# A recurrent attention layer and two expert layers in one kernel: unit 2's outputs, a third hidden bank and wider products in the opening

## The reference

```python
for t in range(S):                     # per batch and head
    m_new = max(f[t] + m, i[t])
    C = exp(f[t] + m - m_new) * C + exp(i[t] - m_new) * outer(v[t], k[t])
    n = exp(f[t] + m - m_new) * n + exp(i[t] - m_new) * k[t]
    y[t] = sigmoid(o[t]) * (C @ q[t]) / max(abs(n @ q[t]), 1)
x = y as 1536 x 320
h = x @ w_in                           # 320 x 2048
g = where(h >= 1, h, where(h <= -1, 0, (h + 1)**2 / 4))
x = g @ w_out                          # 2048 x 320
P = softmax-like gate of x @ w_gate, 8 rounds of row and column scaling
out = sum over 8 experts e of P[:, e] * (max(x @ w1[e], 0) @ w2[e])
```

## Time and profile before

| | |
|---|---|
| median of 3 runs | 923.47 us (922.88 to 923.96) |
| the profiled execution | 923.94 us, of which its span 921.8 us |
| TensorE, matmul busy | 914.6 us, 99% |
| VectorE, ScalarE, GpSimd busy | 594.1, 464.6, 617.8 us |
| granted clock of TensorE, mean | 1.000 |

### The profile page before, as it was taken

The page is one execution under the profiler, slowest core; times in us unless marked ns, Lnnn a source line. Parts: engine busy times, 40 slices in busy tenths (PEclk is TensorE's granted clock), DMA queues, the critical chain, the costliest instruction groups (busy, mean ns, idle before and its releaser), DMA issues.

```text
span 921.8 us, 16392 instructions
## 1 busy us (share of the span) xinstructions
PE 914.6 (99%) x6091; PEld 902.2 (98%) x6091; DVE 594.1 (64%) x1130; ACT 464.6 (50%) x951; POOL 617.8 (67%) x642
## 2 busy tenths in 40 slices
PE   9999999999999999999999999999999999999998
PEld 7899999999999999999999999999999999999998
DVE  7665444447867888866666666666666666666665
ACT  4655545448864445454444445444445444445442
POOL 6963555454786666777777677767776777777652
PEclk9999999999999999999999999999999999999999
DMA  8904324001110111111111111111111111111102
GB/s 263 302 27 115 93 61 104 32 2 38 38 54 22 38 38 38 38 39 59 38 53 38 38 38 38 49 51 44 46 38 38 39 38 60 38 52 38 38 1 86
DMA packets 27599, 53.02 MB, mean 58 GB/s; under 512 B 2304, under 2 KB 15584, under 8 KB 27264
## 3 DMA queue, kind: packets, MB, share of 16 engines
q1 hardware_dynamic: 25984, 46.13, 17.2%
q10 hardware_dynamic: 1440, 5.77, 1.6%
q0 software_dynamic: 96, 0.07, 0.0%
HBM read 49.92 MB, written 2.04 MB: 56 GB/s over the span
## 4 chain that ended last, share of the span: by engine, by line
PE 64%; DVE 1%; issue 0%; ACT 0%; DVEq 0%
PE bank L1680 33%; PE bank L1657 30%; DVE acc L1291 0%; DVE prob L1262 0%; DVE rowsum L1260 0%; DVE prob L1272 0%; DVE h_lo L1308 0%; DVE c L1327 0%; DVE c L1317 0%; DVE acc L1295 0%; ACT h_hi L703 0%; PE bank L1628 0%; ACT h_hi L698 0%; DVE rowinv L1261 0%; DVE colinv L1270 0%
## 5 line engine op out<-in xcount | busy, mean ns | idle before, releaser
L1657 PE MATMUL bank<-xo,wu 128*128 128x384 f32 (+1 forms) x1792 | 377.5, 338 | 0.7 <-DVE s L1311 0.5
L1657 PEld LDWEIGHTS bank<-xo,wu 128*128 128x128 f32 (+1 forms) x1792 | 306.6, 188 | 1.4 <-DVE s L1311 0.7
L1295 DVE SCALAR_TENSOR_TENSOR acc<-bank,prob,acc 128x320 f32<-128x320 f32 x336 | 184.6, 549 | 143.2 <-PE bank L1680 141.7
L1680 PE MATMUL bank<-wd_hi,h_hi 128*128 128x320 f32 x768 | 232.7, 311 | 0.9 <-POOL h_lo L754 0.9
L1680 PE MATMUL bank<-wd_lo,h_hi 128*128 128x320 f32 x768 | 231.3, 309 | 0.0
L754 POOL TENSOR_TENSOR h_lo<-r,h_hi 128x384 fp32r<-128x384 f32 x192 | 194.3, 1031 | 53.2 <-ACT r L704 53.1
L754 POOL TENSOR_TENSOR wu<-raw_up,wu 128x512 fp32r<-128x512 f32 (+1 forms) x128 | 145.6, 1168 | 104.0 <-ACT wu L500 98.7
L703 ACT ACTIVATE h_hi<-c 128x384 fp32r<-128x384 f32 x192 | 100.3, 523 | 185.2 <-DVE c L1317 141.8
L1680 PE MATMUL bank<-wd_hi,h_lo 128*128 128x320 f32 x768 | 174.9, 309 | 0.0
L1680 PEld LDWEIGHTS bank<-wd_hi,h_hi 128*128 128x128 f32 x768 | 144.7, 188 | 1.0 <-issue 0.9
L1680 PEld LDWEIGHTS bank<-wd_lo,h_hi 128*128 128x128 f32 x768 | 145.0, 189 | 0.0
(11 more groups left out here) (154 smaller groups left out, 1307.6 us busy)
## 6 DMA issues: line engine op xcount, KB each, us to landing
raw_up<-ups SPq DMA_DIRECT2D x32, 512.0 KB, 3.5
raw_down<-downs SPq DMA_DIRECT2D x32, 320.0 KB, 2.9
rw<-rows SPq DMA_DIRECT2D x11, 480.0 KB, 6.9
qk_s<-qk SPq DMA_DIRECT2D x12, 416.0 KB
fb<-factors SPq DMA_DIRECT2D x8, 512.0 KB, 6.1
m_raw<-up_down ACTq DMA_DIRECT2D x2, 1440.0 KB, 11.1
result<-acc SPq DMA_DIRECT2D x12, 160.0 KB, 1.9
decb<-factors SPq DMA_DIRECT2D x18, 80.0 KB
```

The costliest lines, as they stand in the source:

```text
L1295: ins = stt(acc[:, unit, :], bank_, prob[:, unit, ex:ex + 1], acc[:, unit, :], ALU.mult, ALU.add)
L1657: last = mm(ring_bank(q, b), a, m, start=(i == 0 and k in (0, 1, 4)), stop=(i == len(parts) - 1), skip_group_check=True)
L1680: last = mm(ps_t[n % RING][:, 0:DM], h[half + f][:, cols], w_[w][:, f, :], start=(i == 0), stop=(i == len(parts) - 1))
```

## The change

- Fillings: 4 become 2 and 2 become 1 in the opening.
- Units 0 and 1 (`heads` with past=False): each weights-by-values product moves the values of two heads, 84 columns, starting anew; the next product overwrites the second head's columns with its own.
- Unit 2: outputs all on VectorE (`last_outputs`): gate times numerator in PSUM, denominator, quotient, and the repeated columns. GpSimd's `over_den(0, 2)` and ScalarE's `twice(2, 2)` go. TensorE waits for `last_twice`.
- VectorE in the opening: `last_decays(2)` moves to f=3, `decays(1, 0, 1)` to f=1, and the three `turn_lo` come ahead of `add_state` and `decays(1, 0, 0)`.
- Bank 2 (`ps_o`) holds the hidden features of f=2, g=0; the wait for `lo1` begins at f=3 instead of f=2; unit 3's scores follow f=2 instead of f=0, its `weigh` is at f=3, and its `heads` waits for `lo1` 3.
- Late columns: bank 0 instead of 2, after f=4 instead of f=1; VectorE copies them at f=5.
- ScalarE's pieces 4 to 9 are made one each at f=1 to f=6; GpSimd takes 4 to 7 at f=2 as before, 8 at f=5 and 9 at f=6.

```diff
-LATE = {0: (4,), 1: (5,), 2: (6, 7), 3: (8,), 4: (9,), 7: (10, 11), 8: (12,), 9: (13,), 12: (14,), 13: (15,)}
+LATE = {1: (4,), 2: (5,), 3: (6,), 4: (7,), 5: (8,), 6: (9,), 7: (10, 11), 8: (12,), 9: (13,), 12: (14,), 13: (15,)}
...
-    ps_late = bank[2]
+    ps_late = bank[0]
...
+    def hidden_bank(g, f):
+        return ps_o if (g, f) == (0, 2) else ps_h[f % 2]
...
-            twice(2, 2)
...
-            over_den(0, 2)
...
-                            if ga == 1 and i == 0:
+                            if ga == 1 and i == 1:
                                 pool.wait_ge(dE_ready, 2)
                             decay_state(ga, i)
...
-                for q in ((4, 5, 6, 7) if f == 2 else LATE.get(f, ())):
+                if f == 2:
+                    pieces = range(TABLES // 2, TABLES)
+                else:
+                    pieces = [q for q in LATE.get(f, ()) if q >= TABLES]
+                for q in pieces:
                     mlp_piece(q)
...
+            def last_outputs(o):
+                i = GT - 1
+                h = o[:, 0:WO].rearrange("p (h d) -> p h d", h=H)
+                dve.wait_ge(heads_out, GT)
+                nc.vector.tensor_scalar(den[:, i, :], h[:, :, D], -1.0, 1.0, ALU.mult, ALU.max).then_inc(den_step, 1)
+                dve.wait_ge(sigmoid_ready, GT)
+                tt(h[:, :, 0:D], h[:, :, 0:D], rw[:, i, 2, :].rearrange("p (h d) -> p h d", h=H), ALU.mult).then_inc(og_r_ready, 1)
+                dve.wait_ge(den_step, 2 * GT - 1)
+                stt(den[:, i, :], h[:, :, D], 1.0, den[:, i, :], ALU.mult, ALU.max).then_inc(den_step, 1)
+                dve.wait_ge(den_step, 2 * GT)
+                nc.vector.reciprocal(rden[:, i, :], den[:, i, :]).then_inc(rden_ready, 1)
+                dve.wait_ge(rden_ready, GT)
+                dve.wait_ge(og_r_ready, GT)
+                tt(xs[:, i, 0:DM].rearrange("p (h d) -> p h d", h=H), h[:, :, 0:D],
+                   rden[:, i, :].unsqueeze(2).to_broadcast([P, H, D]), ALU.mult).then_inc(xs_ready, 1)
+                dve.wait_ge(xs_ready, GT)
+                nc.vector.tensor_copy(xs[:, i, DM:3 * P], xs[:, i, 2 * P:DM]).then_inc(last_twice, 1)
...
             outputs(0, 1, ps_o_of[1])
-            last_decays(2)
-            denominators(0, 2, ps_o_of[2])
+            last_outputs(ps_o_of[2])
+            turn_lo(xa_hi, 0, ps_turn_of[0], 0, xa_ready)
+            turn_lo(xa_hi, 1, ps_turn_of[1], P, xa_ready)
+            turn_lo(xa_hi, 2, ps_turn_of[2], 2 * P, xa_ready)
+            add_state(0, 2, ps_o_of[2])
             dve.wait_ge(fb_made, 4)
             dve.wait_ge(vd_ready, 3)
             decays(1, 0, 0, spread(3, 0))
-            outputs(0, 2, ps_o_of[2])
-            turn_lo(xa_hi, 0, ps_turn_of[0], 0, xa_ready)
-            turn_lo(xa_hi, 1, ps_turn_of[1], P, xa_ready)
-            add_state(0, 2, ps_o_of[2])
-            turn_lo(xa_hi, 2, ps_turn_of[2], 2 * P, xa_ready)
-            decays(1, 0, 1, spread(3, 1))
...
+                    if first and f == UNIT:
+                        decay_columns(2, ps_late_dE[:, 2 * GH:U * H])
+                        gate_columns(2, ps_late)
...
-                    if attention and i < GT and r == 2:
-                        if first and f == 2:
-                            decay_columns(2, ps_late_dE[:, 2 * GH:U * H])
-                            gate_columns(2, ps_late)
+                    if first and f == 1:
+                        decays(1, 0, 1, spread(3, 1))
+                    if first and f == 3:
+                        last_decays(2)
+                    if attention and i < GT and (f == 3 if first and i == 0 else r == 2):
                         weigh(g + 1, i, 0)
                         weigh(g + 1, i, 1)
...
-                        last = mm(o[:, h * DV:(h + 1) * DV], at[:, s, j, a * P:(a + 1) * P], vi[:, i, h, :],
-                                  start=False, stop=True, skip_group_check=True)
+                        n = 1 if past else min(2, H - h)
+                        last = mm(o[:, h * DV:(h + n) * DV], at[:, s, j, a * P:(a + 1) * P],
+                                  vi[:, i, h:h + n, :].rearrange("p h d -> p (h d)"),
+                                  start=not past, stop=True, skip_group_check=True)
...
-            keep_busy(ps_o_of[1], 4)
+            keep_busy(ps_o_of[1], 2)
...
-            keep_busy(ps_o_of[2], 2)
+            keep_busy(ps_o_of[2], 1)
...
-                        if first and f >= 2:
+                        if first and f >= 3:
                             pe.wait_ge(lo1, f - 1)
...
-                        if first and f == 1:
+                        if first and f == 2:
+                            pe.wait_ge(wt_ready, 2 * GT + 2)
+                            weights(g + 1, 0)
+                        if first and f == 4:
+                            pe.wait_ge(at_ready, 2 * GT + 2)
                             late_columns()
-                        if r == 0:
-                            if first and i == 0:
-                                pe.wait_ge(wt_ready, 2 * GT + 2)
+                        if r == 0 and not (first and i == 0):
+                            if first and i == 1:
+                                pe.wait_ge(iT_ready, len(PARTS))
                             weights(g + 1, i)
                         if r == 3:
                             pe.wait_ge(xa_ready, after(g * GT + (GT + i - 1)))
                             if first and i == 0:
-                                pe.wait_ge(dE_ready, 2)
+                                pe.wait_ge(lo1, 3)
                             heads(g + 1, i, ps_o)
```

More of the change, by code:

```diff
@@ L247, in build @@
     ps_decb = bank[7]
-    ps_late = bank[2]
-    ps_late_dE = bank[2][0:QR, P:P + U * H]
+    ps_late = bank[0]
+    ps_late_dE = bank[0][0:QR, P:P + U * H]
     ps_turn_of = (bank[5], bank[3], bank[4])
@@ L257, in build @@
     ps_t = bank[3:6]
+    def hidden_bank(g, f):
+        return ps_o if (g, f) == (0, 2) else ps_h[f % 2]
     def activated(g, f):
-        return ps_h[f % 2][:, 0:GN] if g == 0 else gact[:, f % 2, :]
+        return hidden_bank(g, f)[:, 0:GN] if g == 0 else gact[:, f % 2, :]
     def ring_bank(q, i):
@@ L276, in build @@
     late_gate_in = mk("late_gate_in")
+    last_twice = mk("last_twice")
     fb_in = [mk(f"fb_in{i}") for i in range(GT)]
@@ L639, in mlp @@
                             act.wait_ge(g1, s - 1)
-                        nc.scalar.activation(vhalf[:, f % 2, :], ps_h[f % 2][:, 0:GN], ACT.Relu,
+                        nc.scalar.activation(vhalf[:, f % 2, :], hidden_bank(g, f)[:, 0:GN], ACT.Relu,
                                              bias=0.5, scale=0.5).then_inc(raised, 1)
@@ L917, in mlp_piece_at @@
             def mlp_piece_at(f):
-                if f < 2:
-                    return
-                for q in ((4, 5, 6, 7) if f == 2 else LATE.get(f, ())):
+                if f == 2:
[3 more added lines that the diff above has]
+                for q in pieces:
                     mlp_piece(q)
@@ L1203, in mlp @@
                         dve.wait_ge(sq1, s + 1)
-                        stt(activated(g, f), ps_h[f % 2][:, 0:GN], 1.0, vhalf[:, f % 2, :], ALU.max, ALU.min).then_inc(g1, 1)
+                        stt(activated(g, f), hidden_bank(g, f)[:, 0:GN], 1.0, vhalf[:, f % 2, :], ALU.max, ALU.min).then_inc(g1, 1)
                     extra(f)
@@ L1454, in heads @@
                         h = j * HH + a
-                        last = mm(o[:, h * DV:(h + 1) * DV], at[:, s, j, a * P:(a + 1) * P], vi[:, i, h, :],
-                                  start=False, stop=True, skip_group_check=True)
+                        n = 1 if past else min(2, H - h)
+                        last = mm(o[:, h * DV:(h + n) * DV], at[:, s, j, a * P:(a + 1) * P],
+                                  vi[:, i, h:h + n, :].rearrange("p h d -> p (h d)"),
+                                  start=not past, stop=True, skip_group_check=True)
                 last.then_inc(heads_out, 1)
             def turn_unit(ga, i, dst):
-                pe.wait_ge(x_twice, ga * GT + i + 1)
+                u = ga * GT + i
+                if u == GT - 1:
+                    pe.wait_ge(last_twice, 1)
+                else:
+                    pe.wait_ge(x_twice, u + 1 if u < GT - 1 else u)
                 turn_x(i, dst, xa_turned)
@@ L1588, in mlp @@
                             pe.wait_ge(g1, s - 1)
-                        first_product(ps_h[f % 2], f, m_hi, m_lo, m_st, g * GN, wait_x_lo).then_inc(h1, 1)
+                        first_product(hidden_bank(g, f), f, m_hi, m_lo, m_st, g * GN, wait_x_lo).then_inc(h1, 1)
                     if f == 0 and not first:
```

## The result

On one chip the changed kernel takes 933.63 us (median of 4 runs, 932.95 to 934.77) against 923.21 for the kernel before (4 runs, 922.88 to 923.96). The ratio is 1.0103, 95% interval 1.0078 to 1.0127. It is slower, as forecast, but by 10.4 us instead of 4.2 to 4.5, and beyond the forecast's range (926.2 to 930.2). In the profiled executions the span grew from 921.8 to 931.8 us, and the page has TensorE busy for 917.8 us, 3.2 more than in the earlier trace rows although it makes three fillings fewer: part of the loss is idle time, part is matmuls that ran slower.

What follows compares the result with a forecast made beforehand. TensorE, busy 914.6 of 921.8 us, bounds the kernel. At f=5, -0.89 + 0.24 - 0.8 + 1.75 - 0.25 + 4.1 = 4.15, +4.2 us: 927.7 against the median 923.47, uncertain 926.9 to 928.6; range with rivals 926.2 to 930.2.

Steps and rivals of the forecast that it cites:

- the late piece: Ahead of f=5: GpSimd waits for ScalarE's piece 7, delaying unit 3's decayed state and `add_state`; TensorE idles 4.1 us.
- the heads' hole: Ahead of unit 3's `heads(1, 0)`: TensorE ready at 37.1, begins at 38.85, a new idle of 1.75 us.
- chain to `weigh`: ScalarE's sigmoid, piece 5 and hi 2 to 36.0, then VectorE's lo 2, `last_decays(2)` and two `weigh` to 38.7.
- the copy: Opening, VectorE's copy of 64 columns for unit 2: about 0.15 us, with unit 2's outputs done at 25.2.
- The nearest rival: Opening: unit 2 turned as late as before, held by ScalarE's copies or VectorE's chain; 929.2 us, chance 0.05.
- the clock: Rival: clock falls in the new 4.1 us hole, costing 1.2 us or twice that; 928.9 to 930.1, chance 0.28.
- The earlier trace was the wrong row: Evidence against a clock fall: from 918.0 to the end, 2.9 us of TensorE idleness kept the clock at 1.00.
- The 84 columns: Units 0 and 1, wider weights-by-values products in the opening: 0.24 us more.
- the estimate beside it: Opening: one 2.4 GHz cycle per added column in 28 of 32 products gives 0.49 us, 0.25 above the sum's term.
- the lower of the forecast's bounds: Products of 84 columns cost nothing if the load of the weights sets the pace; the other bound was 0.35 us.
- The fillings: Opening: three fillings fewer, two at 14.38 (0.56 us) and one at 20.26 (0.33), gain 0.89 us.
- the slower cases: Chances: sum as it stands 0.53, clock's fall 0.28, stall partly there 0.07, opening without gain 0.05; slower given as 0.92.

Runs made afterwards that it cites:

- run 3: Changed kernel with GpSimd taking pieces 4 and 5 at f=2, piece 6 at f=3 and piece 7 at f=4: 931.26 us.
- run 1: Changed kernel with unit 2's repeat of 64 columns copied by ScalarE instead of VectorE: 935.44 us.
- run 6: Changed kernel with unit 2's repeated columns made by a second VectorE product out of PSUM instead of a copy within SBUF: 934.62 us.
- run 2: Changed kernel with GpSimd waiting for the end of unit 2's copy, which stays on VectorE, before its decayed state of unit 2: 936.84 us.
- run 5: Changed kernel with 15 fillings instead of 3 ahead of unit 2's turning and 18 more behind the late columns, ahead of f=5: 930.69 us.
- run 4: Changed kernel with 15 fillings instead of 3 ahead of unit 2's turning: 931.9 us.
- run 10: Kernel before with only the products of 84 columns and the three fillings fewer: 923.53 us (10 runs).
- run 9: Kernel before, unchanged, profiled again: 923.47 us.

## Why the prediction was right or wrong

**Right: the late piece.** GpSimd idle 5.90 us ahead of its eighth m_lo (some 5 forecast), released by ScalarE's st_hi; `add_state` 5.48 us late (over 5), released by st_d; TensorE idle 4.17 us ahead of f=5 (4.1). Run 3 removes exactly that hole by the order alone.

**Right in size, by luck in part: the heads' hole**, 1.63 us for 1.75, released by `at`. The forecast's chain to `weigh` left out that unit 3's load must have landed before the sigmoid. With the first layer as early as forecast, that wait exists (1.59 and 1.19 us, runs 1 and 6, released by the load's DMA) and the hole is 3.3 to 3.4. In the changed kernel the late copy covered it.

**Wrong: the copy.** The step that failed is the one that put the repeat at "about 0.15 us" and had unit 2's outputs "done at 25.2". Alone it measures 0.20 (run 2); beside GpSimd's decayed state and pieces, which the change left in place, 3.57. So unit 2 was turned 2.2 us later instead of 1.45 earlier, and the first layer began at 30.73 instead of 27.05: 3.7 us of miss. Runs 1 and 2, whose clock rose nearly as late (6.21 and 6.58), begin it at 27.42 and 27.31, so 3.3 to 3.4 of that is the copy's and the rest mostly the opening's late start. The nearest rival (unit 2 turned as late as before, chance 0.05) blamed VectorE's chain or ScalarE's copies and stopped at 929.2; that two engines may not work on SBUF side by side was not considered, although a copy with both ends in SBUF was the one new kind of instruction in this chain. A sign of it stood in the earlier trace rows: `last_decays(2)`, 16x64 elements, took 0.97 us where 128x320 out of PSUM took 0.47, and the forecast took the 0.97 for its own length.

**Wrong: the clock.** The fall was a rival with a chance of 0.28 and a price of 1.2 us, or twice that. It came twice, once in a hole that the forecast didn't have, and costs 2.8 us by run 5's steps. From the table of the changed kernel alone, the second fall is 10.88 - 9.38 = 1.5. The first is about 1.3: between f=0 and f=3 the late columns, moved out, should give 0.57 back, and 0.72 was lost. The price per fall was about right, the chance too low. The earlier trace rows was the wrong row to lean on, since it ends with the span. Past the span's end the same trace has a granted clock of 0.58 over 921.8 to 924.0: the clock did fall in that idleness, some 0.4 us after the row ends. The page "TensorE: Matmul & The Clock Gate" of the Trainium skill warned of long idle gaps, and was right here: each of the ten holes of 3.0 us or more in these traces had a fall with it.

**Small terms.** The 84 columns cost 0.00 for 0.24, and not the 0.49 of the estimate beside it either; the lower of the forecast's bounds was right. The fillings can't be told from 0.4 to 0.9 (0.89 forecast). The chances of the slower cases add up to 0.93, not 0.92.

**The account.** At f=5 the forecast had +4.15 and the trace has +9.38. The late first layer makes 3.7 of the difference and the first fall 1.3; 0.2 is left over, spread. Behind f=5 come 1.5 for the second fall. The wait of 0.87 us in the expert stage, in the one profile and not in the other, belongs to neither the forecast nor the change: 4.15 + 3.7 + 1.3 + 0.2 + 1.5 - 0.87 = 10.0.

## What to carry to other kernels

When a step changes engine, look at where its operands lie and what GpSimd does at that moment: a VectorE copy within SBUF cost 0.20 us alone and 3.57 beside GpSimd, and the same values by a product out of PSUM cost 0.24. When one chain is pulled forward, walk every list behind it, loads included, and move what it now outruns: of the three late links here (copy, load, piece 7) curing the copy or piece 7 alone left the span between 929.5 and 935.0, curing all gave 919.7. And price a new hole on TensorE at its length plus what the clock may take behind it, 1.3 to 1.5 us a fall here.

## What the runs showed of the hardware that was not expected

- **VectorE kept out over several GpSimd instructions.** In the changed kernel the copy lay from 25.88 to 29.45 while GpSimd took one instruction after another without idle time. It didn't get in at the change from one to the next (27.59, 28.00), but just after the last one before GpSimd had to wait (29.36). In run 2 it was likewise 41.48, just after 41.37. In run 6 it was 39.03, at the one place where GpSimd's next piece wasn't there yet (m_st at 38.91, ScalarE's st_hi of that piece from 38.70 to 39.09). In the kernel before, `last_decays(2)` ended at 24.52, just after 24.41, and GpSimd's next instruction waited until 25.12. Why the changes between are passed over is not shown.
- **A hole puts the clock at risk; its length doesn't settle it.** The ten holes of 3.01 to 5.04 us, in the changed kernel and runs 1 to 4 and 6, each had a fall with them. One of 1.6 ahead of unit 3's heads kept the clock in the changed kernel and in runs 4 and 5, and was followed by a fall at 46 in run 3. The profiled execution of run 10 lost it behind a hole of 1.41 (0.69 over 28:30, 0.50 over 30:32), and run 9 kept it over one of 0.75. The fall itself came anywhere from 2.3 us before a hole's end (run 2, 40.71 against 43.05) to 2.6 behind it (run 3, 45.92 against 43.36). Whether run 10 lost less to the clock than the kernel before because of its edit is open.
